# The second MLP's activation computed as clamp, square and maximum instead of ramp, bend and maximum

## The chip, the cores and the metric

The kernel runs on one core of a Trainium2 chip. The metric is the device time of one launch in microseconds (us). The kernel before took 1396.45 us, the median of 3 runs (1395.6 to 1396.55).

## What is computed

Three stages follow one another on 12288 tokens of width 128. An attention over 768 pooled keys gives `x`; a first MLP with 2048 hidden units and a leaky ReLU follows; then a second MLP of the same size, whose activation is

```python
h = x @ w_in
g = np.where(h >= 1, h, np.where(h <= -1, 0.0, (h + 1) ** 2 / 4))
return g @ w_out
```

Only the way in which this last curve is evaluated differs between the two kernels. Between -1 and 1 the curve is a parabola that lies above `h`; outside it is `max(h, 0)`.

## The kernel before, in words

The tokens are cut into 24 blocks of 512 columns (`NB`, `TB`). Everything is held transposed, so a block is a 128x512 tile. Each matrix product runs with both factors split into a high and a low part in the type fp32r, and so takes three matmuls (`product`, L484 to L488: low weights by high data, high by high, high by low). Each activation is therefore followed by a pair of instructions: ScalarE copies the value to a high part, and VectorE or GpSimd subtracts that from the value and writes the low part.

Iteration `j` of the main loop runs three blocks side by side: the attention of block `j + 1`, the first MLP of block `j` and the second MLP of block `j - 1`. It is cut into 16 slots `s`, one for each group of 128 hidden units. The body is written once per engine, and each engine runs its own list in program order, held back only by semaphores. Iterations 2 to 21 are a hardware loop, the others are unrolled. Iteration 0 has no second MLP, iterations 1 to 22 have all three parts, iteration 23 has no attention, and iteration 24 (the tail) has the second MLP alone. The output of the last block is copied out in iteration 25.

In a slot TensorE issues (L563 to L640): the three matmuls of `mlp1_in(s)` into one of two PSUM banks `h1`; the three of `mlp2_in(s)` into one of two banks `h2`; in slots 0, 2, 4 and 6 the scores of a group `t = s / 2` of 128 queries (`score`, six matmuls); in slots 9 to 14 four transposes of the probabilities (`transpose(k)`, k = 0 to 5) and in slots 10 to 15 the products with the values; then `mlp1_out(s - 2)` and `mlp2_out(s - 3)`. A slot without attention has 12 matmuls.

Three of its waits matter below. The scores of all `t` share one buffer in PSUM, so `score(t)` for t of 1 or more waits until the exponential of `t - 1` has read it (L494). `transpose(0)` waits for the last normalised probabilities (L503), and `transpose(k)` waits until `transposed_lo(k - 1)` has emptied the transposes' buffer (L505).

The second MLP's curve is computed in the ring `g2` of four tiles in SBUF (one quarter each of the array `stage5`; the profile calls it `stage`). The steps of slot `s` are:

- ScalarE, `ramp` (L351): `relu(0.5 h + 0.5)` from PSUM to `g2`.
- VectorE, `bend` (L445): `min(r, 1) * r` on `g2`, in place.
- VectorE, `above` (L451): the maximum of `h` (PSUM) and `g2`, which also frees the PSUM bank.
- ScalarE, `g2_high` (L329), one slot later: the high part.
- GpSimd (L267): the low part, for `mlp2_out`.

Around them ScalarE runs, in order in a slot: `g1_hi` (L342, the first MLP's ReLU), the ramp, `transposed_hi` (L293, slots 9 to 14), the exponential (L283, slots 1, 3, 5, 7), `g2_high(s - 1)`, and `normalise` (L288, slots 2, 4, 6, 8). VectorE runs `g1_lo` (L458), the bend, the maximum, in the slots of an exponential two small instructions on its sum (L381, L386), in the slots of a score the row maximum (L377; in slot 0 it stands ahead of the bend), and `transposed_lo` (L390, slots 9 to 14). At the end of an iteration come `x2_hi` (L369, ScalarE) and `x2_lo` (L477, VectorE), which the next iteration's `mlp2_in(0)` needs.

The exponential's slot in the code of ScalarE:

```python
for s in range(FC):
    ...
    if do.mlp2:
        ...
        act.wait_ge(h2_ready, n + 1)
        ...
    if do.attend and s in EXP_SLOT:
        exponentials(j + 1, EXP_SLOT[s])
    if do.mlp2 and s > 0:
        g2_high(s - 1)
```

Of the kernel before, what the change touches and what calls it, by code (L numbers as in the profile page):

```python
# [23 lines left out]
ACT = mybir.ActivationFunctionType  # L24
# [10 lines left out]
FC = FF // P  # L35
# [3 lines left out]
RING = 4  # L39
# [41 lines left out]
def build(nc, qT, kvT, w_sr, w1_in, w1_inT, w1_out, w2_in, w2_out, outT):  # L81
    ctx = ExitStack()
    with ctx:
# [3 lines left out]
        def sem(name):  # L87
            return ctx.enter_context(nc.semaphore(name))
# [68 lines left out]
        def buffers(a):  # L157
# [29 lines left out]

        h1_ready, g1_hi_done, g1_split, g1_used = (
            sem("h1_ready"), sem("g1_hi_done"), sem("g1_split"), sem("g1_used"))
        h2_ready, ramp_done, bent_done, g2_done, g2_hi_done, g2_split, g2_used = (  # L190
            sem("h2_ready"), sem("ramp_done"), sem("bent_done"), sem("g2_done"),
            sem("g2_hi_done"), sem("g2_split"), sem("g2_used"))

        block = ctx.enter_context(nc.Block())
# [80 lines left out]
        @block.scalar  # L275
        def _(act):
            def split_queries(a):
                act.wait_ge(q_loaded, 16 * (a + 1))
                nc.scalar.activation(q_hi[:], q_raw[:], ACT.Copy).then_inc(q_hi_done, 1)

            def exponentials(a, t):
                act.wait_ge(max_ready, SUB * a + t + 1)
                nc.scalar.activation(probs[t][:], scores_of(a, t), ACT.Exp, bias=neg_max[:, t:t + 1],  # L283
                                     accum_out=exp_sum[:, t:t + 1]).then_inc(exp_done, 1)

            def normalise(a, t):
                act.wait_ge(inv_ready, SUB * a + t + 1)
                nc.scalar.activation(probs[t][:], probs[t][:], ACT.Copy,  # L288
                                     scale=inv_sum[:, t:t + 1]).then_inc(probs_ready, 1)

            def transposed_hi(a, k):
                act.wait_ge(probsT_ready, KC * a + k + 1)
                nc.scalar.activation(pT_hi[k][:], probsT_of(a, k), ACT.Copy).then_inc(pT_hi_done, 1)  # L293

            def attended_hi(a):
                act.wait_ge(x_ready, a + 1)
                nc.scalar.activation(x_hi[:], x_sum, ACT.Copy).then_inc(x_hi_done, 1)

            split_queries(0)

            for k in range(KC):
                ks = slice(k * P, (k + 1) * P)
                act.wait_ge(kv_projected, k + 1)
                nc.scalar.activation(kT_hi[:, ks], kT_sum[k % 2], ACT.Copy, scale=POOL_MEAN * SM_SCALE)
                nc.scalar.activation(v_hi[:, ks], v_sum[k % 2], ACT.Copy, scale=POOL_MEAN).then_inc(kv_hi_done, 1)
            for t in range(SUB):
                exponentials(0, t)
            normalise(0, 0)
            for k in range(KC):
                transposed_hi(0, k)  # L310
            act.wait_ge(lin_ready, 1)
            nc.scalar.activation(lin_hi[:], lin_sum, ACT.Copy, scale=LEAK / (1.0 - LEAK)).then_inc(lin_hi_done, 1)
            split_queries(1)

            def split_w1_in(n):
                ns = slice(n * FF // QUARTERS, (n + 1) * FF // QUARTERS)
                act.wait_ge(w1i_loaded, 16)
                nc.scalar.activation(w1i_hi[:, ns], W1I_RAW[:, ns], ACT.Copy).then_inc(w1i_hi_done, 1)

            split_w1_in(0)  # L320
            attended_hi(0)

            def iteration(j, do):
                def g2_high(s):
                    n = (j - 1) * FC + s
                    act.wait_ge(g2_done, n + 1)
                    if not (isinstance(j, int) and n < RING):
                        act.wait_ge(g2_used, n - RING + 1)
                    nc.scalar.activation(g2_hi[s % RING][:], g2[s % RING], ACT.Copy).then_inc(g2_hi_done, 1)  # L329

                for s in range(FC):
                    if do.mlp2_end and s == LAG2:
                        act.wait_ge(g2_used, FC * (j - 1))
                        if not (isinstance(j, int) and j < 3):
                            act.wait_ge(out_stored, 16 * (j - 2))
                        nc.scalar.activation(out_sb, sum2, ACT.Copy).then_inc(out_copied, 1)
                    if do.mlp1:
                        n = j * FC + s
                        act.wait_ge(h1_ready, n + 1)
                        if not (isinstance(j, int) and n < RING):  # L340
                            act.wait_ge(g1_used, n - RING + 1)
                        nc.scalar.activation(g1_hi[s % RING][:], h1[s % HBANKS], ACT.Relu).then_inc(g1_hi_done, 1)  # L342
                    if do.attend and s == FC - 1:
                        attended_hi(j + 1)
                    if do.mlp2:

                        n = (j - 1) * FC + s
                        act.wait_ge(h2_ready, n + 1)
                        if not (isinstance(j, int) and n < RING):
                            act.wait_ge(g2_split, n - RING + 1)  # L350
                        nc.scalar.activation(g2[s % RING], h2_banks(do)[s % len(h2_banks(do))], ACT.Relu, bias=0.5,  # L351
                                             scale=0.5).then_inc(ramp_done, 1)
                    if do.attend and s in TRANSPOSE_SLOT:
                        transposed_hi(j + 1, TRANSPOSE_SLOT[s])
                    if do.attend and s in EXP_SLOT:
                        exponentials(j + 1, EXP_SLOT[s])
                    if do.mlp2 and s > 0:
                        g2_high(s - 1)
                    if do.attend and s in NORMALISE_SLOT:
                        normalise(j + 1, NORMALISE_SLOT[s])  # L360
                    if do.split_q and s == SPLIT_Q_SLOT:
                        split_queries(j + 2)
                    if isinstance(j, int) and j == 0 and s < QUARTERS - 1:
                        split_w1_in(s + 1)
                if do.mlp2:
                    g2_high(FC - 1)
                if do.mlp1:
                    act.wait_ge(g1_used, FC * (j + 1))
                    nc.scalar.activation(x2_hi[:], sum1, ACT.Copy, scale=1.0 - LEAK).then_inc(x2_hi_done, 1)  # L369

            every_iteration(act, iteration)

        @block.vector
        def _(dve):
# [64 lines left out]
            attended_lo(0)  # L439

            def iteration(j, do):
                def bend(s):

                    dve.wait_ge(ramp_done, (j - 1) * FC + s + 1)
                    nc.vector.scalar_tensor_tensor(g2[s % RING], g2[s % RING], 1.0, g2[s % RING],  # L445
                                                   ALU.min, ALU.mult).then_inc(bent_done, 1)

                def above(s):

                    dve.wait_ge(bent_done, (j - 1) * FC + s + 1)  # L450
                    nc.vector.tensor_tensor(g2[s % RING], h2_banks(do)[s % len(h2_banks(do))], g2[s % RING],  # L451
                                            ALU.max).then_inc(g2_done, 1)

                for s in range(FC):
                    if do.mlp1:

                        dve.wait_ge(g1_hi_done, j * FC + s + 1)
                        nc.vector.scalar_tensor_tensor(g1_lo[s % RING][:], h1[s % HBANKS], 0.0,  # L458
                                                       g1_hi[s % RING][:].bitcast(F32),
                                                       ALU.max, ALU.subtract).then_inc(g1_split, 1)  # L460
                    if do.attend and s == 0:
                        row_max(j + 1, 0)
                    if do.attend and s == FC - 1:
                        attended_lo(j + 1)
                    if do.mlp2:
                        bend(s)
                        above(s)
                    if do.attend and s in EXP_SLOT:
                        guard_sum(j + 1, EXP_SLOT[s])
                        invert_sum(j + 1, EXP_SLOT[s])  # L470
                    if do.attend and s > 0 and s in SCORE_SLOT:
                        row_max(j + 1, SCORE_SLOT[s])
                    if do.attend and s in TRANSPOSE_SLOT:
                        transposed_lo(j + 1, TRANSPOSE_SLOT[s])
                if do.mlp1:
                    dve.wait_ge(x2_hi_done, j + 1)
                    nc.vector.scalar_tensor_tensor(x2_lo[:], sum1, 1.0 - LEAK, x2_hi[:].bitcast(F32),  # L477
# [190 lines left out]
```

## Time and profile before

| what | value |
|---|---|
| median of 3 runs | 1396.45 us |
| span of the profiled execution, first to last instruction | 1394.2 us |
| TensorE busy | 1368.8 us (98%), 6320 matmuls |
| VectorE busy | 1035.5 us (74%), 1660 instructions |
| ScalarE busy | 950.9 us (68%), 1695 instructions |
| GpSimd busy | 563.7 us (40%), 424 instructions |
| granted TensorE clock | 1.000 (2.4 GHz) over the whole span |

The profile records one execution; the page gives its span and no separate time for it. The span lies 2.25 us under the median of the runs, which is the launch's share before the first and after the last instruction. Busy shares are means over stages that differ: a start of some 50 us, the steady iterations, and a tail of 35 us. In the tables below PE is TensorE's matmuls, PEld its weight loads, DVE VectorE, ACT ScalarE, POOL GpSimd. A duration is from an instruction's start to its end; instructions of one engine may overlap by some tens of ns.

### The profile page before, as it was taken

The numbers are of one execution on the slowest core, as the hardware profiler recorded it, in microseconds if no ns is written. First come the engines' busy times: TensorE is split into PE (matmuls) and PEld (weight loads), VectorE is DVE, ScalarE is ACT, GpSimd is POOL, SyncE is SP. The second block draws the span as 40 slices with busy tenths as digits, with TensorE's granted clock in tenths as the row PEclk, the third lists the DMA queues.
The fourth block names the chain that finished last, engine by engine and source line by source line (L and its number), as shares of the span: only waits on it lengthen the run. The fifth ranks groups of instructions, "written<-read, shape, count | busy, mean of one in ns | idle before, by whom it ended". The sixth has DMA issues, their size and how long they took to land.

```text
span 1394.2 us, 21088 instructions
## 1 busy us (share of the span) xinstructions
PE 1368.8 (98%) x6320; PEld 1115.3 (80%) x6320; DVE 1035.5 (74%) x1660; ACT 950.9 (68%) x1695; POOL 563.7 (40%) x424
## 2 busy tenths in 40 slices
PE   5999999999999999999999999999999999999997
PEld 4788888888888888888888888888888888888884
DVE  6577777777777777777787777777877777777777
ACT  3676776766767667677676676776766767667665
POOL 2534344334334344343434434344334334344346
PEclk9999999999999999999999999999999999999999
DMA  8000000000000000000000000000000000000000
GB/s 348 16 0 8 9 15 8 8 15 8 8 8 8 15 8 8 15 2 13 8 8 15 8 8 8 8 15 8 8 15 8 8 8 8 15 0 9 8 1 16
DMA packets 9525, 24.44 MB, mean 18 GB/s; under 512 B 1057, under 2 KB 1185, under 8 KB 8865
## 3 DMA queue, kind: packets, MB, share of 16 engines
q1 hardware_dynamic: 9504, 24.19, 4.9%
q8 instruction: 11, 0.18, 0.1%
q14 instruction: 10, 0.07, 0.0%
HBM read 17.89 MB, written 6.29 MB: 17 GB/s over the span
## 4 chain that ended last, share of the span: by engine, by line
PE 95%; DVE 3%; DMA 1%; ACT 0%; issue 0%; SPq 0%; POOL 0%; POOLq 0%
PE sums L487 13%; PE sums L488 13%; PE sums L486 13%; PE hidden L486 13%; PE hidden L488 13%; PE hidden L487 13%; PE attn L488 5%; PE attn L486 5%; PE attn L487 5%; PE attn L507 4%; DVE stage L445 1%; DVE stage L451 1%; DVE probs L411 1%; DMA stage<-kvT 1%; DVE neg_max L377 0%; PE hidden L507 0%
## 5 line engine op out<-in xcount | busy, mean ns | idle before, releaser
L267 POOL TENSOR_TENSOR g_lo<-stage,g_hi 128x512 fp32r<-128x512 f32 x384 | 508.6, 1324 | 790.4 <-ACT g_hi L329 790.3
L458 DVE SCALAR_TENSOR_TENSOR g_lo<-hidden,g_hi 128x512 fp32r<-128x512 f32 x384 | 265.4, 691 | 265.8 <-ACT g_hi L342 264.3
L342 ACT ACTIVATE g_hi<-hidden 128x512 fp32r<-128x512 f32 x384 | 230.0, 599 | 281.1 <-PE hidden L488 271.8
L445 DVE SCALAR_TENSOR_TENSOR stage<-stage 128x512 f32<-128x512 f32 x384 | 270.9, 705 | 23.1 <-ACT stage L351 21.4
L351 ACT ACTIVATE stage<-hidden 128x512 f32<-128x512 f32 x384 | 230.1, 599 | 74.1 <-PE hidden L488 42.6
L451 DVE TENSOR_TENSOR stage<-hidden,stage 128x512 f32<-128x512 f32 x384 | 265.5, 691 | 13.1
L329 ACT ACTIVATE g_hi<-stage 128x512 fp32r<-128x512 f32 x384 | 242.1, 630 | 31.7 <-DVE stage L451 31.6
L486 PE MATMUL sums<-g_hi,w2o_lo 128*128 128x512 f32 x384 | 152.8, 398 | 4.4 <-POOL g_lo L267 2.8
L486 PE MATMUL hidden<-x_hi,w1i_lo 128*128 128x512 f32 x384 | 152.0, 396 | 1.5 <-DVE x_lo L395 1.5
L486 PE MATMUL sums<-g_hi,w1o_lo 128*128 128x512 f32 x384 | 153.3, 399 | 0.0
L488 PE MATMUL sums<-g_lo,w2o_hi 128*128 128x512 f32 x384 | 151.7, 395 | 0.0
L487 PE MATMUL hidden<-x_hi,w1i_hi 128*128 128x512 f32 x384 | 151.7, 395 | 0.0
L488 PE MATMUL hidden<-x_lo,w2i_hi 128*128 128x512 f32 x384 | 151.7, 395 | 0.0
L486 PE MATMUL hidden<-x_hi,w2i_lo 128*128 128x512 f32 x384 | 151.5, 395 | 0.1
L487 PE MATMUL sums<-g_hi,w2o_hi 128*128 128x512 f32 x384 | 151.6, 395 | 0.0
L487 PE MATMUL sums<-g_hi,w1o_hi 128*128 128x512 f32 x384 | 151.5, 395 | 0.0
L488 PE MATMUL hidden<-x_lo,w1i_hi 128*128 128x512 f32 x384 | 151.2, 394 | 0.0
L488 PE MATMUL sums<-g_lo,w1o_hi 128*128 128x512 f32 x384 | 151.2, 394 | 0.0
L487 PE MATMUL hidden<-x_hi,w2i_hi 128*128 128x512 f32 x384 | 150.7, 392 | 0.0
L486 PEld LDWEIGHTS sums<-g_hi,w2o_lo 128*128 128x128 f32 x384 | 72.2, 188 | 26.1 <-POOL g_lo L267 9.2
L390 DVE TENSOR_TENSOR pT_lo<-attn,pT_hi 128x512 fp32r<-128x512 f32 x135 | 91.8, 680 | 0.1
L486 PEld LDWEIGHTS hidden<-x_hi,w1i_lo 128*128 128x128 f32 x384 | 72.3, 188 | 19.0 <-issue 1.9
(107 smaller groups left out, 2090.2 us busy)
## 6 DMA issues: line engine op xcount, KB each, us to landing
q_raw<-qT SPq DMA_DIRECT2D x24, 256.0 KB, 2.7
stage<-kvT SPq DMA_DIRECT2D x12, 512.0 KB, 8.8
outT<-stage SPq DMA_DIRECT2D x24, 256.0 KB, 2.0
stage<-w_out SPq DMA_DIRECT2D x2, 1024.0 KB, 14.1
stage<-w_in SPq DMA_DIRECT2D x2, 1024.0 KB, 14.1
stage<-w_inT SPq DMA_DIRECT2D x1, 1024.0 KB, 13.9
probs<-w_sr SPq DMA_DIRECT2D x1, 64.0 KB, 1.9
```

The costliest lines, as they stand in the source:

```text
L267: nc.gpsimd.tensor_tensor(g2_lo[s % RING][:], g2[s % RING], g2_hi[s % RING][:].bitcast(F32), ALU.subtract).then_inc(g2_split, 1)
L329: nc.scalar.activation(g2_hi[s % RING][:], g2[s % RING], ACT.Copy).then_inc(g2_hi_done, 1)
L342: nc.scalar.activation(g1_hi[s % RING][:], h1[s % HBANKS], ACT.Relu).then_inc(g1_hi_done, 1)
L351: nc.scalar.activation(g2[s % RING], h2_banks(do)[s % len(h2_banks(do))], ACT.Relu, bias=0.5, scale=0.5).then_inc(ramp_done, 1)
L390: nc.vector.tensor_tensor(pT_lo[k][:], probsT_of(a, k), pT_hi[k][:].bitcast(F32), ALU.subtract).then_inc(pT_split, 1)
L445: nc.vector.scalar_tensor_tensor(g2[s % RING], g2[s % RING], 1.0, g2[s % RING], ALU.min, ALU.mult).then_inc(bent_done, 1)
L451: nc.vector.tensor_tensor(g2[s % RING], h2_banks(do)[s % len(h2_banks(do))], g2[s % RING], ALU.max).then_inc(g2_done, 1)
L458: nc.vector.scalar_tensor_tensor(g1_lo[s % RING][:], h1[s % HBANKS], 0.0, g1_hi[s % RING][:].bitcast(F32), ALU.max, ALU.subtract).then_inc ...
L486: nc.tensor.matmul(out, w_lo, m_hi, start=start, stop=False)
L487: nc.tensor.matmul(out, w_hi, m_hi, start=False, stop=False)
L488: return nc.tensor.matmul(out, w_hi, m_lo, start=False, stop=stop)
L507: last = nc.tensor.transpose(probsT_of(a, k)[:, t * P:(t + 1) * P], probs[t][:, k * P:(k + 1) * P], ident[:])
```

## The change

The same curve is taken from a clamped input: with `c = min(max(h, -1), 1)`, `g = max(h, (0.5 c + 0.5)^2)`. The steps of slot `s` become:

- VectorE, `clamp` (L446 of the changed kernel): both bounds in one instruction, from PSUM to `g2`.
- ScalarE, the square (L350): `(0.5 c + 0.5)^2` on `g2`, in place.
- VectorE, `above` (L452): as before, but moved to the head of slot `s + 1`, ahead of `g1_lo(s + 1)`; in the tail it follows `clamp(s + 1)`.
- ScalarE, `g2_high(s)`: in slot `s + 1`, now ahead of the square of that slot and so ahead of the exponential; in the tail it stays behind it.

The wait for `h2_ready` and that for the ring (`g2_split`) move from ScalarE to VectorE. TensorE, GpSimd and SyncE keep their lists.

```diff
# ScalarE
-                        act.wait_ge(h2_ready, n + 1)
-                        if not (isinstance(j, int) and n < RING):
-                            act.wait_ge(g2_split, n - RING + 1)
-                        nc.scalar.activation(g2[s % RING], h2_banks(do)[s % len(h2_banks(do))], ACT.Relu, bias=0.5,
-                                             scale=0.5).then_inc(ramp_done, 1)
+                        if do.mlp1 and s > 0:
+                            g2_high(s - 1)
+                        act.wait_ge(clamped, (j - 1) * FC + s + 1)
+                        nc.scalar.activation(g2[s % RING], g2[s % RING], ACT.Square, bias=0.5,
+                                             scale=0.5).then_inc(squared, 1)
...
-                    if do.mlp2 and s > 0:
+                    if do.mlp2 and not do.mlp1 and s > 0:
                         g2_high(s - 1)
# VectorE
-                def bend(s):
-
-                    dve.wait_ge(ramp_done, (j - 1) * FC + s + 1)
-                    nc.vector.scalar_tensor_tensor(g2[s % RING], g2[s % RING], 1.0, g2[s % RING],
-                                                   ALU.min, ALU.mult).then_inc(bent_done, 1)
+                def clamp(s):
+                    n = (j - 1) * FC + s
+                    dve.wait_ge(h2_ready, n + 1)
+                    if not (isinstance(j, int) and n < RING):
+                        dve.wait_ge(g2_split, n - RING + 1)
+                    nc.vector.tensor_scalar(g2[s % RING], h2_banks(do)[s % len(h2_banks(do))], -1.0, 1.0,
+                                            ALU.max, ALU.min).then_inc(clamped, 1)
...
                 def above(s):
 
-                    dve.wait_ge(bent_done, (j - 1) * FC + s + 1)
+                    dve.wait_ge(squared, (j - 1) * FC + s + 1)
...
                 for s in range(FC):
+                    if do.mlp1 and do.mlp2 and s > 0:
+                        above(s - 1)
...
                     if do.mlp2:
-                        bend(s)
-                        above(s)
+                        clamp(s)
+                        if not do.mlp1 and s > 0:
+                            above(s - 1)
...
+                if do.mlp2:
+                    above(FC - 1)
                 if do.mlp1:
                     dve.wait_ge(x2_hi_done, j + 1)
```

The order of ScalarE's work in slots 0 and 1 of the loop body (`stage5` is the ring `g2`; ISA and REGISTER_ALU rows set up waits), before:

```order
L342 ACTIVATE g1_hi0<-hidden 128x512 [waits g1_used]
L348 ISA
L350 REGISTER_ALU [waits h2_ready]
L351 ACTIVATE stage5<-hidden 128x512 [waits g2_split]
L339 REGISTER_ALU
L341 REGISTER_ALU [waits h1_ready]
L342 ACTIVATE g1_hi1<-hidden 128x512 [waits g1_used]
L348 REGISTER_ALU
L350 REGISTER_ALU [waits h2_ready]
L351 ACTIVATE stage5<-hidden 128x512 [waits g2_split]
L282 ISA
L283 ACTIVATE probs0,exp_sum<-attn,neg_max 128x768 [waits max_ready]
```

and of the change:

```order
L342 ACTIVATE g1_hi0<-hidden 128x512 [waits g1_used]
L349 ISA
L350 ACTIVATE stage5<-stage5 128x512 [waits clamped]
L339 REGISTER_ALU
L341 REGISTER_ALU [waits h1_ready]
L342 ACTIVATE g1_hi1<-hidden 128x512 [waits g1_used]
L328 REGISTER_ALU [waits g2_done]
L329 ACTIVATE g2_hi0<-stage5 128x512 [waits g2_used]
L349 REGISTER_ALU
L350 ACTIVATE stage5<-stage5 128x512 [waits clamped]
L282 ISA
L283 ACTIVATE probs0,exp_sum<-attn,neg_max 128x768 [waits max_ready]
```

Ahead of the exponential of group 0 (L283) stood the ramp, which waits for TensorE; now `g2_high(0)` and the square stand there, which wait for VectorE.

VectorE in the same two slots, before:

```order
L458 SCALAR_TENSOR_TENSOR g1_lo0<-hidden,g1_hi0 128x512 [waits g1_hi_done]
L376 ISA
L377 TENSOR_REDUCE neg_max<-attn 128x1 [waits scores_ready]
L444 ISA
L445 SCALAR_TENSOR_TENSOR stage5<-stage5 128x512 [waits ramp_done]
L451 TENSOR_TENSOR stage5<-hidden,stage5 128x512 [waits bent_done]
L457 REGISTER_ALU
L458 SCALAR_TENSOR_TENSOR g1_lo1<-hidden,g1_hi1 128x512 [waits g1_hi_done]
```

and of the change:

```order
L461 SCALAR_TENSOR_TENSOR g1_lo0<-hidden,g1_hi0 128x512 [waits g1_hi_done]
L375 ISA
L376 TENSOR_REDUCE neg_max<-attn 128x1 [waits scores_ready]
L443 ISA
L445 REGISTER_ALU [waits h2_ready]
L446 TENSOR_SCALAR stage5<-hidden 128x512 [waits g2_split]
L452 TENSOR_TENSOR stage5<-hidden,stage5 128x512 [waits squared]
L460 REGISTER_ALU
L461 SCALAR_TENSOR_TENSOR g1_lo1<-hidden,g1_hi1 128x512 [waits g1_hi_done]
```

The maximum of slot 0 still stands ahead of `g1_lo` of slot 1, but between it and the clamp lies now a step of ScalarE.

## Rows read from the trace of the kernel before

**Rows 1.** The page, part 4: the chain that ended last, by engine.

```profile
PE 95%; DVE 3%; DMA 1%; ACT 0%; issue 0%; SPq 0%; POOL 0%; POOLq 0%
```

**Rows 2.** Windows: steady part and tail; start:end, length, busy us and count of each engine, PEclk, DMA share, GB/s.

```profile
76.50:1358.50 1282.00, 1281.93 (x5924) 1049.03 (x5924) 960.51 (x1544) 894.52 (x1587) 511.41 (x389) 1.00 0.03 9
1359.50:1394.20 34.70, 27.18 (x100) 17.35 (x99) 26.31 (x33) 19.20 (x34) 22.23 (x16) 1.00 0.04 16
```

**Rows 3.** Groups of VectorE by form: busy us, mean ns, idle before and its releaser.

```profile
L445 DVE SCALAR_TENSOR_TENSOR stage<-stage 128x512 f32<-128x512 f32 x384 | 270.9, 705 | 23.1 <-ACT stage L351 21.4
...
L458 DVE SCALAR_TENSOR_TENSOR g_lo<-hidden,g_hi 128x512 fp32r<-128x512 f32 x384 | 265.4, 691 | 265.8 <-ACT g_hi L342 264.3
...
L423 DVE TENSOR_SCALAR probs<-probs,inv_sum 128x768 f32<-128x768 f32 x3 | 1.8, 612 | 0.0
```

**Rows 4.** The same view, ScalarE: the exponential and its accumulator read.

```profile
L283 ACT ACTIVATE probs<-attn,neg_max 128x768 f32<-128x768 f32 x91 | 81.8, 899 | 2.2 <-DVE neg_max L377 2.2
...
L283 ACT ACTIVATION_READ_ACCUMULATOR probs<-attn,neg_max 128x1 f32 x91 | 18.2, 200 | 0.0
```

**Rows 5.** Timeline, slots 0 to 2 of one iteration: start us, duration us, engine, instruction.

```profile
414.06 0.39 PE L488 MATMUL hidden<-x_lo,w2i_hi 128*128 128x512 f32 x1
...
414.56 0.60 ACT L351 ACTIVATE stage<-hidden 128x512 f32<-128x512 f32 x1 [1.84 <-PE hidden L488]
...
416.45 0.90 ACT L283 ACTIVATE probs<-attn,neg_max 128x768 f32<-128x768 f32 x1
...
417.24 0.20 ACT L283 ACTIVATION_READ_ACCUMULATOR probs<-attn,neg_max 128x1 f32 x1
...
417.77 0.39 PE L486 MATMUL attn<-kT_hi,q_lo 128*128 128x512 f32 x1
```

**Rows 6.** Timeline, slots 3 to 10 of the same iteration.

```profile
421.37 0.39 PE L488 MATMUL hidden<-x_lo,w1i_hi 128*128 128x512 f32 x1
...
425.09 0.39 PE L486 MATMUL attn<-kT_hi,q_lo 128*128 128x512 f32 x1
...
428.00 0.39 PE L488 MATMUL hidden<-x_lo,w1i_hi 128*128 128x512 f32 x1
...
431.71 0.40 PE L486 MATMUL attn<-kT_hi,q_lo 128*128 128x512 f32 x1
...
434.63 0.39 PE L488 MATMUL hidden<-x_lo,w1i_hi 128*128 128x512 f32 x1
...
439.55 0.93 ACT L288 ACTIVATE probs<-probs,inv_sum 128x768 f32<-128x768 f32 x1
...
441.13 0.60 PE L507 MATMUL attn<-ident,probs 128*128 128x128 f32 x4
...
444.35 0.60 PE L507 MATMUL attn<-ident,probs 128*128 128x128 f32 x4
```

**Rows 7.** Waits of TensorE's weight loads, 76 to 1358 us: total us, times, longest.

```profile
PEld attn L486 <- ACT probs L283: 0.3, 1, 0.3
```

**Rows 8.** Timeline of the tail, one row or two each of VectorE, ScalarE, GpSimd, TensorE.

```profile
1358.82 0.69 DVE L477 SCALAR_TENSOR_TENSOR x_lo<-sums,x_hi 128x512 fp32r<-128x512 f32 x1 [1.37 <-ACT x_hi L369]
...
1361.92 0.69 DVE L451 TENSOR_TENSOR stage<-hidden,stage 128x512 f32<-128x512 f32 x1
...
1362.53 0.68 DVE L445 SCALAR_TENSOR_TENSOR stage<-stage 128x512 f32<-128x512 f32 x1
...
1362.65 0.63 ACT L329 ACTIVATE g_hi<-stage 128x512 fp32r<-128x512 f32 x1 [0.78 <-DVE stage L451]
...
1366.66 1.39 POOL L267 TENSOR_TENSOR g_lo<-stage,g_hi 128x512 fp32r<-128x512 f32 x1 [0.32 <-ACT g_hi L329]
...
1367.53 1.07 DVE L445 SCALAR_TENSOR_TENSOR stage<-stage 128x512 f32<-128x512 f32 x1
...
1388.78 1.27 POOL L267 TENSOR_TENSOR g_lo<-stage,g_hi 128x512 fp32r<-128x512 f32 x1 [0.33 <-ACT g_hi L329]
...
1390.11 0.51 PE L486 MATMUL sums<-g_hi,w2o_lo 128*128 128x512 f32 x1 [0.65 <-POOL g_lo L267]
```

More of the change, by code:

```diff
@@ L189, in build @@
             sem("h1_ready"), sem("g1_hi_done"), sem("g1_split"), sem("g1_used"))
-        h2_ready, ramp_done, bent_done, g2_done, g2_hi_done, g2_split, g2_used = (
-            sem("h2_ready"), sem("ramp_done"), sem("bent_done"), sem("g2_done"),
+        h2_ready, clamped, squared, g2_done, g2_hi_done, g2_split, g2_used = (
+            sem("h2_ready"), sem("clamped"), sem("squared"), sem("g2_done"),
             sem("g2_hi_done"), sem("g2_split"), sem("g2_used"))
@@ L345, in iteration @@
                     if do.mlp2:
-                        n = (j - 1) * FC + s
-                        act.wait_ge(h2_ready, n + 1)
-                        if not (isinstance(j, int) and n < RING):
-                            act.wait_ge(g2_split, n - RING + 1)
-                        nc.scalar.activation(g2[s % RING], h2_banks(do)[s % len(h2_banks(do))], ACT.Relu, bias=0.5,
-                                             scale=0.5).then_inc(ramp_done, 1)
+                        if do.mlp1 and s > 0:
[3 more added lines that the diff above has]
+                                             scale=0.5).then_inc(squared, 1)
                     if do.attend and s in TRANSPOSE_SLOT:
```

## The prediction, made before the changed kernel ran

> **What bounds the kernel now.** I read first the chain that ended last: TensorE holds 95% of it [rows 1]. The windows then separate two regimes. From 76.5 to 1358.5 us TensorE is busy 1281.93 of 1282.00 us at clock 1.00 (2.4 GHz): it waits for nothing, so no saving on another engine can shorten this part, and any new wait of TensorE lengthens it. In the tail it is busy only 27.18 of 34.70 us [rows 2]. So the change can win in the tail alone, and the question for the steady part is how much room each thing has that TensorE waits for. The timeline gives that room; I read it at every `score` and `transpose`, and it is smallest at `score(1)`. In slot 1 the exponential starts at 416.45, its accumulator read ends at 417.24 + 0.20 = 417.44, and TensorE starts `score(1)`, which waits for it, at 417.77 [rows 5]; the weight load of that matmul leads it by one matmul's spacing (0.23, below), so some 0.1 us is left. That this wait is real shows once: the only wait of TensorE's weight loads for the exponential in this stretch is 0.3 us long [rows 7], in iteration 1, where the first slots are shorter.
>
> Matmul spacing: from `score(2)` at 425.09 to `score(3)` at 431.71 there are 24 products of 512 columns and a score (3 long, 3 half as long) [rows 6]; 6.62 / 28.5 gives 0.232 us.
>
> **Prices.** The clamp is a VectorE instruction 128x512 from PSUM. `g1_lo`, which also reads PSUM, takes 0.691 [rows 3]; I take 0.69. The trace has no such TENSOR_SCALAR from PSUM. The nearest of its kind, from SBUF, takes 0.612 for 768 columns [rows 3]; scaled by columns that is 0.41, and as it has a fixed part too I put the low end at 0.46. Nothing of 512 columns on this engine takes more than 0.705 undisturbed. I take 0.69 because clamp and `g1_lo` share the source memory. The Trainium skill, VectorE: DVE Perf Modes, section "Why PSUM operands drop a tier", says that an fp32 operand in PSUM excludes the double rate that an SBUF one may get, which speaks against the low end; its table in "The TRN2 errata" would give (120 + 512) / 0.96 GHz = 0.658 us, an estimate by which the sum below would be about 5 us smaller.
> The square is a ScalarE instruction from SBUF: 0.63, as `g2_high` [rows 8]. Hand-over from one engine to the next is 0.03 to 0.04 (maximum of 1361.92 ends 1362.61, `g2_high` starts 1362.65). VectorE starts the next independent instruction 0.61 after the last one's start (1361.92 to 1362.53) [rows 8]; ScalarE's next after one of 512 columns comes 0.49 to 0.53 later. Exponential with its read: 416.45 to 417.44, 0.99 [rows 5], and the groups of all 91 such exponentials, with means of 0.899 and 0.200, show that they are alike [rows 4]. After a real wait, TensorE's matmul starts 0.06 after the releaser (GpSimd ends 1388.78 + 1.27 = 1390.05, matmul 1390.11) and lasts 0.51 instead of 0.40 [rows 8], so a release at R delays a matmul due at M by R + 0.17 - M.
>
> **Steady iterations: the exponential moves behind a round trip.** Before, what preceded `exp` on ScalarE waited for TensorE alone. Now it waits for the clamp, which waits behind `g1_lo`, which waits for `g1_hi`. Iteration by iteration, times as in the trace before, "late" being TensorE's accumulated delay:
>
> 1. `mlp2_in(0)` ends at 414.06 + 0.39 = 414.45; its reader started 0.11 later, at 414.56 [rows 5]. Clamp(0) 414.56 to 415.25, square(0) to 415.91, maximum(0) from 415.94, `g1_lo(1)` from 416.55, clamp(1) 417.16 to 417.85, square(1) from 417.88, `exp(0)` 0.53 later, 418.41 to 419.40. It ended at 417.44. `score(1)` was due at 417.77: **1.80 late**.
> 2. `mlp1_in(3)` ended at 421.76 [rows 6], now 423.56. From there `g1_hi` (0.04 + 0.60), `g1_lo` (0.03, then 0.61 to the clamp), clamp 0.69, hand-over 0.03, 0.53 of the square: 2.53 in all. `exp(1)` 426.09 to 427.08; `score(2)` due 425.09 + 1.80 = 426.89 [rows 6]: 0.36 more, 2.16.
> 3. `mlp1_in(5)` ended at 428.39 [rows 6], now 430.55; ScalarE is held by `normalise(1)` until 430.70, then 2.49 as above: `exp(2)` 433.19 to 434.18; `score(3)` due 431.71 + 2.16 = 433.87: 0.48 more, 2.64.
> 4. `mlp1_in(7)` ended at 435.02 [rows 6], now 437.66; ScalarE is held by `normalise(2)` until 437.80, `exp(3)` 440.29 to 441.28. `g1_hi(8)` can only start behind it, at 441.18; the two small sum instructions and maximum(7) go first on VectorE (441.31 to 442.28), `g1_lo(8)` starts 442.20, clamp(8) 442.81 to 443.50, square(8) 443.53, `normalise(3)` 444.06 to 444.99 (0.93, rows 6). Before it ended at 440.48. `transpose(0)` was due at 441.13 + 2.64 = 443.77: 1.39 more, 4.03.
> 5. `g1_hi(9)` 444.90, `g1_lo(9)` 445.53, clamp(9) 446.14 to 446.83, square(9) 446.86, `transposed_hi(0)` 447.39, `transposed_lo(0)` 448.01 to 448.69; `transpose(1)` due 444.35 + 4.03 = 448.38: 0.48 more, **4.51 late**.
>
> Slots 10 to 14 last 3.9 us each, longer than the chain, and no further wait follows: `transpose(2)` is due near 452.8, its releaser ends near 452.4. What else moves is covered. `g2_high` and GpSimd's low part come earlier than before; the PSUM banks `h2` are freed 1.5 us later but are wanted two slots on; `x2_lo` would end 0.4 us later and still 0.3 ahead of `mlp2_in(0)`'s weight load. DMAs are untouched. The iterations with attention and second MLP are 1 to 22: 22 x 4.51 = **+99.2 us**. Iteration 23 has no exponential: 0.
>
> **The tail.** Here VectorE paced the kernel: bends took 1.07 instead of 0.68 us whenever they started while GpSimd's subtraction ran (1366.66 to 1368.05) [rows 8]. The Trainium skill, SBUF — State Buffer, section "SBUF: two separate sides", calls the port pair that both use an exclusive lock, taken by a VectorE instruction with two SBUF inputs; the trace agrees, 1.07 against 0.68. Clamp and maximum have at most one SBUF input, so a slot should fall from 1.70 us (13 of them lie between the low parts of 1366.66 and 1388.78) to the six matmuls' 1.39. The start is 0.38 later: `x2_lo`, which ended at 1359.51 [rows 8], now closes a chain with clamp and square. By the prices above the first low part then runs from 1363.75 to 1365.05 and its product starts at 1365.11. Eleven slots later, at 1380.55, TensorE has issued `mlp2_in(15)`, which ends at 1380.70. Clamp(15) takes until 1381.43, maximum(14) until 1382.04, `g2_high(14)` until 1382.70, and the last two low parts of 1.30 until 1385.4. Before, the last ended at 1390.05: **-4.65 us**.
>
> **Sum.** 99.2 - 4.65 = +94.5. On the profiled span of 1394.2 that is 1488.7; the runs' median lies 2.25 above the span, so 1396.45 + 94.5 = **1491 us**.
>
> **The bounds.** Seven clamps lie in the chain of one iteration (2, 1, 1, 2, 1). At 0.46 each, 1.6 us of the 4.51 goes: 22 x 2.9 - 4.65 = +59, 1456 us. Upward, if the hand-overs that need a register instruction first cost 0.11 rather than 0.03, about twelve of them add 1 us an iteration: 1513 us. That case's own range is 1456 to 1515.
>
> **The rivals.**
> - *Faster.* If ScalarE's exponential is not held (the scores had more room than 0.1 us, or the round trip fits in the slot), only the tail counts: 1396.45 - 4.65 = 1392 us. The busy shares of 74 and 68% speak for room on average; the 0.1 us at `score(1)` and the 0.3 us wait [rows 5, 7] speak against. It decides at an exponential ending before 417.5.
> - *Only the first wait.* Once `score(1)` is 1.80 late the helpers have caught up, and scores 2, 3 and the transposes find their data: 22 x 1.80 - 4.65 = +35, 1431 us. Against it: steps 2 and 4 start anew from TensorE's own matmuls.
> - *More waits.* The ring of transposes has only 0.4 us left in slots 10 to 14. If each of the five steps there loses 0.5 us, 2.5 x 22 = +55: 1546 us.
> - *The change does not do what it says*, for instance a reload of ScalarE's table between square and exponential: the lists of both kernels show a single ACT_TABLE_LOAD, at the start, so 1%.
>
> **Chances.** Forecast 0.78, only the first wait 0.08, more waits 0.08, faster 0.05, the last 0.01. The range 1448 to 1522 holds the forecast's bounds with a little for a mix with its neighbours, and leaves out the rivals, some 2 in 10. A measurement of this kernel tells about 0.2% (2.8 us) from no change: slower 0.94, faster 0.05, same 0.01.
>
> **What would show it.** In the profile after: TensorE's waits gain `attn` for the exponential, near 1.8 us at `score(1)` and 0.4 to 0.5 at the next two; 1.4 us for `normalise`; 0.5 for `transposed_lo(0)`; an iteration 4.5 us longer; clamps of 0.69; tail slots of 1.39 us and no VectorE instruction of 1.07 in it. TensorE still at 0.07 us of idleness in the steady part would make the prediction wrong at its root; clamps near 0.46 would shrink it by a third.

## The result, and the profile after

| | before | after |
|---|---|---|
| median | 1396.31 us (4 runs, 1395.60 to 1396.55) | 1489.94 us (4 runs, 1489.04 to 1490.72) |
| ratio | | 1.067, 95% interval 1.0655 to 1.0685 |
| span of the profiled execution | 1394.2 us | 1487.8 us |
| granted TensorE clock | 1.000 | 1.000 |

The change costs 93.6 us; +94.5 was forecast. The parts 1 and 4 of the page of the changed kernel answer to [rows 1]:

```profile
PE 1398.5 (94%) x6320; PEld 1105.8 (74%) x6320; DVE 981.0 (66%) x1660; ACT 958.2 (64%) x1695; POOL 552.0 (37%) x424
...
PE 42%; DVE 22%; issue 17%; ACT 16%; DVEq 1%; ACTq 1%; DMA 1%; SPq 0%; POOL 0%; POOLq 0%
```

TensorE held 95% of the chain that ended last; now it is 42%, and VectorE (22%), ScalarE (16%) and "issue" (17%, time in which an engine waited for nothing that the profile shows) stand in it. VectorE's busy time is lower than before (981 against 1035.5 us) and the kernel is slower all the same: the engines wait for one another in turn. The windows of the steady part and of the tail, with the columns of [rows 2]:

```profile
77.00:1457.00 1380.00, 1314.79 (x5928) 1039.25 (x5927) 911.85 (x1545) 900.69 (x1587) 501.28 (x389) 1.00 0.02 8
1458.00:1487.80 29.80, 24.51 (x99) 18.14 (x99) 20.62 (x32) 20.45 (x34) 20.67 (x17) 1.00 0.05 18
```

The steady part had 0.07 us of idle TensorE; now it has 65.2 of 1380 us, and a wait costs more than its idle time, as the matmuls below show. The tail shrank from 34.7 to 29.8 us. The waits of TensorE's weight loads over the whole span (total us, times, longest), where before only the 0.3 us of [rows 7] stood in the steady part:

```profile
PEld attn L492 <- ACT probs L283: 66.3, 66, 2.2
PEld attn L513 <- ACT probs L288: 31.7, 23, 1.4
PEld attn L513 <- DVE pT_lo L389: 14.7, 22, 0.7
...
PEld attn L492 <- DVE pT_lo L389: 8.6, 22, 0.4
```

66 waits for the exponential are three for each of 22 iterations. 22 each are for `normalise` (one of the 23 is from the start), for `transposed_lo` at the transposes, and for `transposed_lo` at the values; the last was not forecast. A weight load leads its matmul by 0.23 us, so these totals are larger than what TensorE loses; the loss is read from the matmuls below.

The new instructions by form (columns of [rows 3]) show the prices: clamp 0.682, square 0.632.

```profile
L446 DVE TENSOR_SCALAR stage<-hidden 128x512 f32<-128x512 f32 x384 | 261.7, 682 | 4.6 <-PE hidden L494 2.0
...
L350 ACT ACTIVATE stage<-stage 128x512 f32<-128x512 f32 x384 | 242.8, 632 | 301.3 <-DVE stage L446 301.1
```

The timeline of slots 0 to 2 of one iteration (VectorE, then ScalarE, then TensorE) is the counterpart of [rows 5], with times 27.5 us later:

```profile
442.13 0.69 DVE L446 TENSOR_SCALAR stage<-hidden 128x512 f32<-128x512 f32 x1
443.52 0.69 DVE L452 TENSOR_TENSOR stage<-hidden,stage 128x512 f32<-128x512 f32 x1 [0.70 <-ACT stage L350]
444.12 0.68 DVE L461 SCALAR_TENSOR_TENSOR g_lo<-hidden,g_hi 128x512 fp32r<-128x512 f32 x1
444.72 0.68 DVE L446 TENSOR_SCALAR stage<-hidden 128x512 f32<-128x512 f32 x1
...
442.85 0.63 ACT L350 ACTIVATE stage<-stage 128x512 f32<-128x512 f32 x1 [2.50 <-DVE stage L446]
...
445.44 0.63 ACT L350 ACTIVATE stage<-stage 128x512 f32<-128x512 f32 x1 [0.48 <-DVE stage L446]
445.97 0.88 ACT L283 ACTIVATE probs<-attn,neg_max 128x768 f32<-128x768 f32 x1
446.76 0.19 ACT L283 ACTIVATION_READ_ACCUMULATOR probs<-attn,neg_max 128x1 f32 x1
...
445.09 0.40 PE L494 MATMUL hidden<-x_lo,w2i_hi 128*128 128x512 f32 x1
447.00 0.51 PE L492 MATMUL attn<-kT_hi,q_lo 128*128 128x512 f32 x1 [1.51 <-ACT probs L283]
447.34 0.39 PE L493 MATMUL attn<-kT_hi,q_hi 128*128 128x512 f32 x1
```

Read it as one chain: clamp(0) at 442.13, square(0) 442.85, maximum(0) 443.52, `g1_lo(1)` 444.12, clamp(1) 444.72, square(1) 445.44, exponential 445.97 to 446.95 (its read ends there), `score(1)` 447.00. Without a wait `score(1)` would have started 0.23 behind the matmul of 445.09, at 445.32.

### The profile page after: what moved, and what is told of

Its sections match the earlier page's. It is cut to its first block, busy times and chain, and to the rows that moved or that the text cites. A ratio compares the mean times of both kernels' runs of the same rounds, so it can differ in the third digit from the quotient of the medians.

```text
span 1487.8 us, 21088 instructions
## 1 busy us (share of the span) xinstructions
PE 1398.5 (94%) x6320; PEld 1105.8 (74%) x6320; DVE 981.0 (66%) x1660; ACT 958.2 (64%) x1695; POOL 552.0 (37%) x424
## 4 chain that ended last, share of the span: by engine, by line
PE 42%; DVE 22%; issue 17%; ACT 16%; DVEq 1%; ACTq 1%; DMA 1%; SPq 0%; POOL 0%; POOLq 0%
DVE stage L446 10%; PE sums L494 5%; PE sums L492 5%; PE sums L493 5%; DVE g_lo L461 5%; PE hidden L492 4%; PE hidden L494 4%; PE hidden L493 4%; ACT probs L288 4%; ACT probs L283 4%; PE attn L513 4%; PE attn L492 4%; ACT g_hi L342 3%; PE attn L494 3%; PE attn L493 3%
## 5 line engine op out<-in xcount | busy, mean ns | idle before, releaser
L267 POOL TENSOR_TENSOR g_lo<-stage,g_hi 128x512 fp32r<-128x512 f32 x384 | 496.7, 1294 | 895.0 <-ACT g_hi L329 894.0
L350 ACT ACTIVATE stage<-stage 128x512 f32<-128x512 f32 x384 | 242.8, 632 | 301.3 <-DVE stage L446 301.1
L452 DVE TENSOR_TENSOR stage<-hidden,stage 128x512 f32<-128x512 f32 x384 | 261.5, 681 | 57.4 <-ACT stage L350 57.3
L342 ACT ACTIVATE g_hi<-hidden 128x512 fp32r<-128x512 f32 x384 | 226.2, 589 | 91.6 <-PE hidden L494 91.2
L446 DVE TENSOR_SCALAR stage<-hidden 128x512 f32<-128x512 f32 x384 | 261.7, 682 | 4.6 <-PE hidden L494 2.0
L513 PE MATMUL attn<-ident,probs 128*128 128x128 f32 x540 | 83.5, 277 | 27.0 <-ACT probs L288 21.6
L513 PEld LDWEIGHTS attn<-ident,probs 128*128 128x128 f32 x540 | 63.8, 140 | 58.3 <-ACT probs L288 31.7
```

What stands on the lines that cost most here:

```text
L267: nc.gpsimd.tensor_tensor(g2_lo[s % RING][:], g2[s % RING], g2_hi[s % RING][:].bitcast(F32), ALU.subtract).then_inc(g2_split, 1)
L350: nc.scalar.activation(g2[s % RING], g2[s % RING], ACT.Square, bias=0.5, scale=0.5).then_inc(squared, 1)
L446: nc.vector.tensor_scalar(g2[s % RING], h2_banks(do)[s % len(h2_banks(do))], -1.0, 1.0, ALU.max, ALU.min).then_inc(clamped, 1)
L513: last = nc.tensor.transpose(probsT_of(a, k)[:, t * P:(t + 1) * P], probs[t][:, k * P:(k + 1) * P], ident[:])
```

## The experiments

Each was run beside the kernel before, on the same chip. That kernel's median was 1396.3 us beside four of the runs (the exponential ahead of the square, nothing behind the square, the tail alone, the bend from PSUM) and 1396.8 beside the other four, which ran on a second chip. Their edits are shown against the changed kernel, or where it says so against the kernel before. The rival to the theory of the prediction was that the two helper engines' lists are too long as a whole, so that no order of them would do.

### The exponential ahead of the square

```diff
                     if do.attend and s == FC - 1:
                         attended_hi(j + 1)
+                    if do.attend and s in EXP_SLOT:
+                        exponentials(j + 1, EXP_SLOT[s])
                     if do.mlp2:
...
-                    if do.attend and s in EXP_SLOT:
-                        exponentials(j + 1, EXP_SLOT[s])
```

> The changed kernel with one thing moved: on ScalarE the exponential stands directly behind g1_hi, ahead of g2_high and of the square. Theory (the exponential waits behind the round trip g1_lo, clamp, square): the waits at the three scores (1.80, 0.36 and 0.48 us by the prediction, 1.79, 0.34 and 0.40 in the profile after) go, since exp(0) now starts near 415.8, earlier than before the change. normalise(3) and transposed_hi stay behind squares: normalise(3) starts 2.53 after the end of mlp1_in(8) and ends some 0.1 us after transpose(0) is due, so 0.3 us are left there and up to 0.5 at transpose(1): 0.8 us an iteration, 22 x 0.8 = 18, less 4.8 of the tail: about 1410 us (1400 to 1420). Rival (VectorE's and ScalarE's lists are simply too long, wherever the exponential stands): still above 1450 us.

Measured: 1412.63 us, ratio 1.0115 (1.0099 to 1.013). One moved line takes back 77 of the 94 us. The waits of its weight loads:

```profile
PEld attn L513 <- DVE pT_lo L389: 14.6, 22, 0.7
PEld attn L513 <- ACT probs L288: 10.5, 23, 0.6
...
PEld attn L492 <- DVE pT_lo L389: 8.5, 22, 0.4
```

No steady wait for the exponential is left, and the three others stand, the one for `normalise` with at most 0.6 instead of 1.4 us. An iteration, from one `x2_lo` to the next, lasts 57.24 us instead of the 56.33 before the change, so 0.91 more where 0.8 was expected: TensorE loses 0.24 and 0.44 at the first two transposes, a little less than expected, and 0.22 at the values, which was not expected. That is most of the 2.6 us by which the run missed its number.

### Exponential and normalise ahead

```diff
+                    if do.attend and s in EXP_SLOT:
+                        exponentials(j + 1, EXP_SLOT[s])
+                    if do.attend and s in NORMALISE_SLOT:
+                        normalise(j + 1, NORMALISE_SLOT[s])
                     if do.mlp2:
```

(and both removed from their old places)

> Between the runs e1_exp_first and e2_attn_first: exponential and normalise ahead of g2_high and square, transposed_hi still behind the square. Theory: normalise(3) is in time again, and transposed_lo(0), whose chain from the end of mlp1_in(9) (440.99) ends at 444.82 while transpose(1) is due at 444.35, keeps one wait of 0.64 us an iteration: 22 x 0.64 = 14, 1392 + 14 = 1406 us (1402 to 1408). Rival (normalise was all that was left): 1393 us.

Measured: 1401.25 us, ratio 1.0032 (1.002 to 1.0044).

```profile
PEld attn L513 <- DVE pT_lo L389: 8.8, 22, 0.4
PEld attn L492 <- DVE pT_lo L389: 8.7, 22, 0.4
```

Normalise's wait is gone and the two waits for `transposed_lo` are left, as the theory has it. The size was wrong: I had taken the end of `mlp1_in(9)` as 440.99, and the trace before has 440.20 + 0.40 = 440.60:

```profile
440.20 0.40 PE L488 MATMUL hidden<-x_lo,w1i_hi 128*128 128x512 f32 x1
```

From there the chain ends 0.39 earlier, and the wait comes to 0.25 us instead of 0.64. Both waits show 0.4 us at the weight loads, as the one at the values does in the changed kernel, where it costs 0.23; two of 0.2 make 9 us in 22 iterations. The next run, without them, is 8.3 us faster, or 7.8 when each is compared with the kernel before on its own chip.

### Nothing that TensorE waits for behind the square

As the run before, and:

```diff
                         if do.mlp1 and s > 0:
                             g2_high(s - 1)
+                        if do.attend and s in TRANSPOSE_SLOT:
+                            transposed_hi(j + 1, TRANSPOSE_SLOT[s])
                         act.wait_ge(clamped, (j - 1) * FC + s + 1)
```

> As the run before, and also normalise directly behind the exponential's place, ahead of g2_high and the square, and transposed_hi ahead of the square (behind g2_high). Theory: nothing that TensorE waits for stands behind the round trip any more, the steady part is TensorE's own again, and only the tail's gain is left: 1396.4 - 4.7 = 1391.7 us (1390.5 to 1393), faster than both kernels. If transposed_hi, now waiting for TensorE's transposes, holds the square and through it the maximum and g1_lo, some waits of TensorE stay: up to 0.4 us an iteration, 1400 us. Rival (lists too long): above 1420 us.

Measured: 1392.93 us, ratio 0.9974 (0.9964 to 0.9984). The same clamp, square and late maximum, the same number of instructions on every engine, and the kernel is faster than before the change. So the helpers' lists are not too long: the 94 us came from where three kinds of instruction stood on ScalarE. It stays 1.2 us above the sum. Of that 0.4 is the later `x2_lo` at the tail's head and 0.6 is iteration 1, which lasts 55.3 us instead of 54.7; the iterations after it last 56.33 us, as before the change.

### The new curve in the tail alone

Against the kernel before: clamp, square and maximum one slot late only where `do.mlp1` is false.

```diff
-                        bend(s)
-                        above(s)
+                        if do.mlp1:
+                            bend(s)
+                            above(s)
+                        else:
+                            clamp(s)
+                            if s > 0:
+                                above(s - 1)
```

> The kernel before with the new curve in the tail (iteration 24) alone; the steady iterations keep ramp, bend and maximum. Theory: TensorE's steady part unchanged, tail slots of 1.39 instead of 1.70 us: 1396.4 - 5.0 = 1391.4 us (the 0.38 of a later x2_lo at the tail's head does not arise here). Rival (the tail's shorter time in the profile after comes from something else, such as helpers that were ahead): 1396 us.

Measured: 1391.45 us, ratio 0.9966 (0.9952 to 0.9979), 4.9 us under the kernel before; 5.0 were expected. Its median is the lowest of this study, but its interval overlaps that of the run before, so the runs do not tell the two apart.

### The bend with one operand from PSUM

Against the kernel before.

```diff
-                    nc.vector.scalar_tensor_tensor(g2[s % RING], g2[s % RING], 1.0, g2[s % RING],
+                    nc.vector.scalar_tensor_tensor(g2[s % RING], h2_banks(do)[s % len(h2_banks(do))], 1.0, g2[s % RING],
```

> The kernel before, with one operand of the bend read from PSUM instead of SBUF: min(h, 1) * r instead of min(r, 1) * r, so another curve, but the same instructions, order and waits. It has one SBUF input instead of two. Theory (the bend's 1.07 us in the tail is a wait for the port pair that GpSimd holds): bends of 0.69 in the tail, slots of 1.39, and about 1391.5 us (1390.5 to 1393). Rival (VectorE's three dependent steps and their hand-overs, not the port, set 1.70 us a slot): bends of 1.07 stay or the idle moves elsewhere, 1396 us.

Measured: 1391.86 us, ratio 0.9963 (0.9949 to 0.9976). VectorE in its tail, and GpSimd's low parts (13 in one row):

```profile
1366.81 0.69 DVE L445 SCALAR_TENSOR_TENSOR stage<-hidden,stage 128x512 f32<-128x512 f32 x1 [0.34 <-ACT stage L351]
1367.53 0.69 DVE L451 TENSOR_TENSOR stage<-hidden,stage 128x512 f32<-128x512 f32 x1
1368.14 0.68 DVE L445 SCALAR_TENSOR_TENSOR stage<-hidden,stage 128x512 f32<-128x512 f32 x1
...
1368.97 17.14 POOL L267 TENSOR_TENSOR g_lo<-stage,g_hi 128x512 fp32r<-128x512 f32 x13 [0.29 <-ACT g_hi L329]
```

Bends of 0.69 where the kernel before had 1.07 [rows 8], in the same order and with the same semaphores. The low parts follow one another at 1.32 us, and the `mlp2_in` of TensorE's last ten slots start 1.40 apart, where they were 1.70 apart before. In the steady part an iteration stays at 56.33 us in both kernels. So 4.4 of the 4.9 us that the new curve gains in the tail come from one source operand (the two intervals overlap), and the clamp is only one way to get rid of it.

### The kernel before with its exponential one place later

Against the kernel before, the only edit: the exponential behind `g2_high`.

```diff
-                    if do.attend and s in EXP_SLOT:
-                        exponentials(j + 1, EXP_SLOT[s])
                     if do.mlp2 and s > 0:
                         g2_high(s - 1)
+                    if do.attend and s in EXP_SLOT:
+                        exponentials(j + 1, EXP_SLOT[s])
```

> The kernel before with one thing moved: the exponential stands behind g2_high instead of ahead of it, no clamp and no square. It starts about 0.73 us later in slot 1 (behind g2_high(0), which waits for the maximum that ends at 416.61: exp(0) 417.18 to 418.17) and 0.53 later in slots 3 and 5. Theory (score(1) has 0.1 us of room, scores 2 and 3 have 0.9): a wait of 418.17 + 0.17 - 417.77 = 0.57 us at score(1) and none elsewhere, 22 x 0.57 = 12.5: 1409 us. Rival (TensorE has more room at score(1) than the profile shows): 1396 us.

Measured: 1408.50 us, ratio 1.0084 (1.007 to 1.0098), within 0.5 us of the sum. ScalarE and TensorE at `score(1)` of one iteration:

```profile
534.00 0.63 ACT L329 ACTIVATE g_hi<-stage 128x512 fp32r<-128x512 f32 x1
534.54 0.88 ACT L283 ACTIVATE probs<-attn,neg_max 128x768 f32<-128x768 f32 x1
535.32 0.19 ACT L283 ACTIVATION_READ_ACCUMULATOR probs<-attn,neg_max 128x1 f32 x1
...
535.56 0.50 PE L486 MATMUL attn<-kT_hi,q_lo 128*128 128x512 f32 x1 [0.28 <-ACT probs L283]
```

The read of the accumulator ends at 535.51 and the matmul follows at 535.56. The 0.1 us of room at `score(1)` that [rows 5] shows is real, and it alone prices the displaced exponential of this run: an iteration lasts 56.87 instead of 56.33 us.

### Half a clamp more in each slot

```diff
+                    if do.mlp1:
+                        nc.vector.tensor_scalar(spare[s % RING], bank[:, 0:TB // 2], -1.0, 1.0,
+                                                ALU.max, ALU.min)
```

> The changed kernel with one more VectorE instruction in front of each clamp of the steady iterations: a clamp of 256 of the 512 columns into a spare tile. By the rows of the profile (0.14 us for one column, 0.69 for 512) it takes 0.42 us and moves what follows by 0.34. Theory (seven clamps lie one behind another between TensorE's own matmuls in an iteration): 7 x 0.34 = 2.4 us an iteration, 22 x 2.4 = 52, so 1542 us; up to 1560 if transposed_lo in slots 10 to 14, which has 0.4 us left, loses it too. Rival (the delay is ScalarE's and the hand-overs', VectorE with 66% busy has room for 0.34 more a slot): under 1500 us.

Measured: 1598.6 us, the median of three executions (1596.7 to 1601.3), ratio 1.1455 (1.1434 to 1.1476): +109 against the changed kernel, twice the 52 expected. A fourth execution took 2748.2 us; it was not profiled, so what made it so long is not shown. The rival (VectorE has room) falls; the sum was too small. Three matmuls that ended a wait: `transpose(0)`, `values(5)`, and `score(1)` of the next iteration.

```profile
504.56 0.33 PE L518 MATMUL attn<-ident,probs 128*128 128x128 f32 x1 [1.96 <-ACT probs L289]
...
528.57 0.50 PE L497 MATMUL attn<-pT_hi,v_lo 128*128 128x512 f32 x1 [0.54 <-DVE pT_lo L390]
...
542.00 0.50 PE L497 MATMUL attn<-kT_hi,q_lo 128*128 128x512 f32 x1 [2.10 <-ACT probs L284]
```

Idle plus 0.27 (0.22 at a transpose) is the loss. For `transpose(0)`, `transpose(1)`, `values(5)` and scores 1 to 3 it is 2.18, 0.77, 0.81, 2.37, 0.84 and 1.05 us, against 1.21, 0.44, 0.23, 1.79, 0.34 and 0.40 in the changed kernel. That is 3.6 more; with short waits at the four other transposes, which use up the 0.4 us that they had, an iteration grew by 4.2 us (64.9 against 60.7 from `x2_lo` to `x2_lo`). Counting clamps on the path found 2.4 of it, a little over half. My reading of the rest, which no run of its own tests: in slots 5, 7 and 8 ScalarE was already held by an instruction of the slot before (steps 3 and 4 of the prediction), so with less room the delays add up from slot to slot. The 22 iterations make 93 us of the 107 by which the span of the profiled execution grew. Another 11 stand in nine iterations in which the clock fell (below), and 3.5 in iteration 23, which has no attention and lasts 49.5 us instead of 46.0.

### The high part back behind the exponential

```diff
-                        if do.mlp1 and s > 0:
-                            g2_high(s - 1)
...
-                    if do.mlp2 and not do.mlp1 and s > 0:
+                    if do.mlp2 and s > 0:
                         g2_high(s - 1)
```

> The changed kernel with g2_high put back behind the exponential, as in the kernel before. The first wait does not depend on it (1.80 us at score(1), square and exponential unmoved), but g2_high then delays g1_hi of the next slot on ScalarE by about 0.5 us behind each exponential: 0.5 more at score(2) and at transpose(0), perhaps 0.5 at score(3): 1.0 to 1.5 us an iteration, 1512 to 1523 us. Rival (g2_high's new place is what costs the time): below 1490 us. Rival (its place does not matter): 1490 us.

Measured: 1569.13 us, ratio 1.1236 (1.1218 to 1.1253): 79 us more than the changed kernel, where 22 to 33 were expected. The sign tells that `g2_high`'s new place ahead of the square is the half of the reordering that helps. The size was wrong by more than a factor of two. In the iteration from 524 to 589 us TensorE loses 1.78, 0.86, 1.08 and 2.56 us at the three scores and at `transpose(0)`, and 0.23 at the values, 6.5 in all or 2.1 more than the changed kernel, where 1.0 to 1.5 were expected. And the clock fell behind the longest of these waits, which was not expected at all. TensorE's matmul that ended the longest wait, then busy time per engine in stretches of 1 us (PE, PEld, DVE, ACT, POOL, granted clock):

```profile
559.34 0.33 PE L511 MATMUL attn<-ident,probs 128*128 128x128 f32 x1 [2.34 <-ACT probs L288]
...
557.00:558.00 1.00, 0.00 (x0) 0.00 (x0) 0.30 (x2) 0.69 (x2) 0.00 (x0) 1.00 0.00 0
...
560.00:561.00 1.00, 1.00 (x4) 0.75 (x4) 1.00 (x2) 0.00 (x0) 0.00 (x0) 0.60 0.00 0
561.00:562.00 1.00, 1.00 (x3) 0.79 (x3) 0.09 (x1) 0.88 (x2) 0.00 (x0) 0.50 0.00 0
...
563.00:564.00 1.00, 1.00 (x5) 0.82 (x4) 0.56 (x1) 0.40 (x1) 1.00 (x1) 0.69 0.00 0
564.00:565.00 1.00, 1.00 (x8) 0.87 (x7) 0.77 (x2) 0.20 (x1) 0.12 (x1) 1.00 0.00 0
```

TensorE does nothing from the end of its last matmul, 557.00, to 559.34; from 560.2 to 563.6 the granted clock is 0.50 (1.2 GHz). Seventeen such falls of some 3.4 us can be counted in this profile, one each in 17 of the 22 iterations, and the mean clock is 0.981.

The lengths of the iterations price both. An iteration of the changed kernel lasts 60.7 us. Here the four in which the clock did not fall, apart from the shorter iteration 1, last 63.3, and the seventeen in which it fell 64.4. So the waits cost 2.6 us an iteration, 57 in all, and a fall adds 1.1, 19 in all. A fall loses half of 3.4 us of clock, 1.7, but part of that is given back: with TensorE later, the wait at `transpose(1)` goes, and only five of the 22 iterations still have it. The last 4 us are iteration 23, which lasts 50.0 us instead of 46.0. It has no attention and so shorter slots, and TensorE's weight loads wait in it six times for the maximum, once for `g1_lo` (1.4 us) and once for GpSimd's low part (1.9 us), none of which the changed kernel has there.

## Why the prediction was right, step by step

The forecast case came true. Matmuls of TensorE in one iteration of the changed kernel, each time the last ahead of a wait and the one that ended it (`score(2)`, `score(3)`, `transpose(0)`, `transpose(1)`, `values(5)`), are the counterpart of [rows 6]:

```profile
454.20 0.40 PE L494 MATMUL hidden<-x_lo,w2i_hi 128*128 128x512 f32 x1
454.66 0.50 PE L492 MATMUL attn<-kT_hi,q_lo 128*128 128x512 f32 x1
...
461.15 0.40 PE L494 MATMUL hidden<-x_lo,w2i_hi 128*128 128x512 f32 x1
461.67 0.51 PE L492 MATMUL attn<-kT_hi,q_lo 128*128 128x512 f32 x1
...
470.95 0.40 PE L494 MATMUL hidden<-x_lo,w2i_hi 128*128 128x512 f32 x1
472.33 0.33 PE L513 MATMUL attn<-ident,probs 128*128 128x128 f32 x1 [0.99 <-ACT probs L288]
...
475.40 0.40 PE L494 MATMUL hidden<-x_lo,w2i_hi 128*128 128x512 f32 x1
476.01 0.44 PE L513 MATMUL attn<-ident,probs 128*128 128x128 f32 x2 [0.22 <-DVE pT_lo L389]
...
494.77 0.40 PE L494 MATMUL hidden<-x_lo,w1i_hi 128*128 128x512 f32 x1
495.12 0.50 PE L492 MATMUL attn<-pT_hi,v_lo 128*128 128x512 f32 x1
```

A matmul is due 0.23 behind its forerunner; what it starts later, plus 0.11 (0.06 at a transpose) for the slower restart, is the loss.

| wait | predicted us | measured us |
|---|---|---|
| `score(1)` for the exponential | 1.80 | 447.00 - 445.32 + 0.11 = 1.79 |
| `score(2)` | 0.36 | 0.34 |
| `score(3)` | 0.48 | 0.40 |
| `transpose(0)` for `normalise` | 1.39 | 1.21 |
| `transpose(1)` for `transposed_lo` | 0.48 | 0.44 |
| `transpose(2)` | 0 | 480.00, due 480.00: 0 |
| `values(5)` for `transposed_lo` | 0 | 0.23 |
| sum | 4.51 | 4.41 |

- **The price of the clamp** (0.69, low end 0.46): 0.682. The row of the same source memory was the right neighbour; the SBUF form of the instruction was not. By the table of the Trainium skill (VectorE: DVE Perf Modes, "The TRN2 errata") it would be 0.658, an estimate from its PSUM column. The measurement stands nearer to the row of this kernel.
- **The round trip**: right, and shown by undoing it. Moving the exponential alone takes back 77 us, moving all three instructions 97, with nothing removed.
- **A sum right by two errors.** `transpose(0)` came out 0.18 smaller: the chain from the end of `mlp1_in(7)` to the end of `normalise(3)` took 7.21 instead of 7.33 us, as several links were 0.01 to 0.02 shorter, and the other 0.06 is that a transpose restarts faster than a matmul of 512 columns. `values(5)` was missed: in slot 15 the values stand directly behind `mlp1_in(15)`, with neither `mlp2_in(15)` nor a transpose ahead of them. In slots 10 to 14 what waits for `transposed_lo` comes behind `mlp2_in`, three matmuls or 0.7 us later, and the prediction counts 0.4 us of room for it. I had said that no wait follows `transpose(1)`; that was checked for transposes alone. The first error is worth 4 us of the 93.6, the second 5, with opposite signs: that the sum came out within 1 us is luck, that it came out near is not.
- **22 iterations**: the time from the first to the last `x2_lo` grew by 97.8 us (1380.9 against 1283.1), where 99.2 and 0.38 at the end were forecast.
- **The tail**: -4.65 forecast against the span before, of which 0.38 lies ahead of the last `x2_lo`. From that `x2_lo` to the end it is 30.6 us instead of 35.3, so -4.7 where the steps give -5.0. The 0.7 us that are left of the 93.6 lie ahead of the first `x2_lo`. GpSimd's low parts (14 in one row) and VectorE in the tail of the changed kernel, the counterpart of [rows 8]:

```profile
1461.81 2.58 POOL L267 TENSOR_TENSOR g_lo<-stage,g_hi 128x512 fp32r<-128x512 f32 x2 [3.74 <-ACT g_hi L329]
1464.63 19.12 POOL L267 TENSOR_TENSOR g_lo<-stage,g_hi 128x512 fp32r<-128x512 f32 x14 [0.25 <-ACT g_hi L329]
...
1463.47 0.68 DVE L446 TENSOR_SCALAR stage<-hidden 128x512 f32<-128x512 f32 x1
1464.07 0.68 DVE L452 TENSOR_TENSOR stage<-hidden,stage 128x512 f32<-128x512 f32 x1
1465.25 0.69 DVE L446 TENSOR_SCALAR stage<-hidden 128x512 f32<-128x512 f32 x1 [0.50 <-PE hidden L494]
```

No instruction of VectorE lasts 1.07 us, and 19.12 / 14 is 1.37 us a slot against 1.70. At 1465.25 VectorE waits for TensorE: the pace is TensorE's again. Low parts of 1.29 against the 1.39 of [rows 8] show that GpSimd had been slowed as well. By the Trainium skill (SBUF — State Buffer, "SBUF: two separate sides") this is what a lock on the shared port pair gives, and the run with the bend from PSUM agrees. Whether it is a lock or another kind of sharing, the runs do not tell.
- **The rivals**: "only the first wait" and "faster" fall with the waits at scores 2 and 3. "More waits" came in part, as `values(5)`, at 5 us instead of 55. That the middle waits exist although the first one had delayed TensorE confirms that they start anew from TensorE's own matmuls. A reload of ScalarE's table falls too: the trace of the changed kernel holds a single ACT_TABLE_LOAD, at the start, of 1.28 us, as the one before does.

## What to carry to other kernels

When one engine is never idle, ask of every instruction that it waits for how long before its due time it ends, and what stands ahead of it on its engine: here the exponential had 0.1 us of room at one score, and where it stood was worth 77 of the 94 us. A step that hands work to another engine and waits for it is best kept behind the instructions on which the busy engine depends: with those put first, the same round trip left the steady iterations of this kernel at 56.33 us. The VectorE instruction with two SBUF operands beside GpSimd work was worth rewriting where VectorE set the pace, in the tail, and brought nothing in the steady part.

## What the runs showed of the hardware

- **The clock after long waits.** In the changed kernel TensorE is idle for 1.5 us ahead of `score(1)` in an iteration, once for 1.8, and the clock stays at 1.00. With `g2_high` put back it is idle for 2.3 to 2.4 us ahead of `transpose(0)` in every iteration, and in 17 of 22 the clock fell to 0.50 for some 3.4 us behind it; in five it did not, with the same wait. With the extra half clamp it is idle for 2.0 us ahead of `transpose(0)` and 2.1 ahead of `score(1)`, and the clock fell in nine of 22 iterations (mean 0.988). So a wait of a little over 2 us cost more than its own length in some iterations and not in others; I had expected waits to cost their own length only. What decides it no run here shows.
- **Restart.** A 512-column matmul that ends a wait lasts 0.50 to 0.51 instead of 0.39, and the next starts 0.34 instead of 0.23 behind it (447.00 and 447.34 above): 0.11 us for each wait.
- **Same operation, other partners.** ScalarE's `g1_hi` has a mean of 0.589 us in the changed kernel and 0.599 before, the exponential 0.884 and 0.899, with unchanged operands. Why was not tried.
